# One-hot products of the last expert between two expert layers, and ten unread products moved ahead of the router's ranks

## The reference, cut to what matters

```python
# 1. gated linear attention: batch 2, 8 heads, 768 positions, head_dim 40; its output is x: 1536 tokens x 320
# 2. first expert layer: 8 experts, each token goes to its best 2 (320 -> 1024 -> 320, ReLU)
logits = x @ w_gate
noise_scale = np.log1p(np.exp(x @ w_noise))
noisy_logits = logits + noise_scale * noise
top2 = np.argpartition(-noisy_logits, 2, axis=1)[:, :2]
top2_l = np.take_along_axis(noisy_logits, top2, axis=1)
top2_w = np.exp(top2_l - top2_l.max(-1, keepdims=True))
top2_w /= top2_w.sum(-1, keepdims=True) + 1e-09
for e in range(8):
    for k in range(2):
        mask = top2[:, k] == e
        h = np.maximum(x[mask] @ w1[e], 0.0)
        out[mask] += top2_w[mask, k, None] * (h @ w2[e])
# 3. second expert layer: 4 experts, every token goes through all
p = domain_probs / (domain_probs.sum(-1, keepdims=True) + 1e-09)
for e in range(4):
    out += p[:, e:e + 1] * (np.maximum(x @ w1[e], 0.0) @ w2[e])
```

## Time and profile before

| | us |
|---|---|
| device time, median of 3 runs | 715.22 (714.48 to 716.89) |
| device time of the profiled execution | 714.77 |
| its span | 712.9 |
| TensorE busy | 680.1 (95%) |
| VectorE busy | 384.0 (54%) |
| ScalarE busy | 285.3 (40%) |
| GpSimd busy | 102.4 (14%) |

### The profile page before, as it was taken

The page is one execution under the profiler, slowest core; times in us unless marked ns, Lnnn a source line. Parts: engine busy times, 40 slices in busy tenths (PEclk is TensorE's granted clock), DMA queues, the critical chain, the costliest instruction groups (busy, mean ns, idle before and its releaser), DMA issues.

```text
span 712.9 us, 11459 instructions
## 1 busy us (share of the span) xinstructions
PE 680.1 (95%) x4265; PEld 623.2 (87%) x4265; DVE 384.0 (54%) x634; ACT 285.3 (40%) x486; POOL 102.4 (14%) x144
## 2 busy tenths in 40 slices
PE   9999989999999999997389999999999999999997
PEld 7888976999999999997388989888898898898886
DVE  6677764666644754752345545546445554454422
ACT  5545533555443654552143423324334343242311
POOL 7433202522022020000512002011100001000000
PEclk9999999999999999999599999999999999999999
DMA  6347551755544758711473425234243253332001
GB/s 226 113 112 191 192 171 38 224 164 156 168 138 128 203 156 309 265 37 39 134 225 114 130 67 166 88 111 148 88 128 88 74 146 108 108 98 65 0 0 37
DMA packets 28665, 91.85 MB, mean 129 GB/s; under 512 B 4656, under 2 KB 10800, under 8 KB 28624
## 3 DMA queue, kind: packets, MB, share of 16 engines
q1 hardware_dynamic: 21328, 75.57, 35.2%
q0 software_dynamic: 3072, 10.49, 5.1%
q10 hardware_dynamic: 4224, 5.24, 2.0%
HBM read 76.87 MB, written 14.42 MB: 128 GB/s over the span
## 4 chain that ended last, share of the span: by engine, by line
PE 91%; DVE 3%; issue 2%; DMA 2%; ACT 1%; POOL 1%; DVEq 0%; ACTq 0%; POOLq 0%
PE pY L1270 13%; PE pY L1272 13%; PE pY L1271 12%; PE pH L1255 10%; PE pH L1256 9%; PE pH L1257 9%; PE pH L1262 5%; PE pH L1260 5%; PE psYa L1142 3%; PE psD L1057 2%; PE pH L1206 2%; PE pT L1232 1%; PE psS L1077 1%; PE psYa L1162 1%; DVE PM L760 1%
## 5 line engine op out<-in xcount | busy, mean ns | idle before, releaser
L626 ACT ACTIVATE h_hi<-pH 128x512 fp32r<-128x512 f32 x160 | 95.7, 598 | 273.8 <-PE pH L1262 268.6
L947 DVE SCALAR_TENSOR_TENSOR h_lo<-pH,h_hi 128x512 fp32r<-128x512 f32 x160 | 110.5, 691 | 164.1 <-ACT h_hi L626 160.2
L1270 PE MATMUL pY<-w_hi,h_hi 128*128 128x320 f32 x608 | 189.0, 311 | 2.3 <-DVE h_lo L947 1.7
L1272 PE MATMUL pY<-w_hi,h_lo 128*128 128x320 f32 x608 | 187.5, 308 | 0.0
L1271 PE MATMUL pY<-w_lo,h_hi 128*128 128x320 f32 x608 | 187.5, 308 | 0.0
L1255 PE MATMUL pH<-x_hi,w_hi 128*128 128x512 f32 (+3 forms) x324 | 123.8, 382 | 3.7 <-issue 2.3
L746 DVE TENSOR_TENSOR w_lo<-stage,w_hi 128x1024 fp32r<-128x1024 f32 (+1 forms) x80 | 108.5, 1358 | 28.0 <-ACT w_hi L553 27.8
L1270 PEld LDWEIGHTS pY<-w_hi,h_hi 128*128 128x128 f32 x608 | 114.1, 188 | 10.4 <-issue 5.3
L1256 PE MATMUL pH<-x_lo,w_hi 128*128 128x512 f32 (+3 forms) x324 | 120.8, 373 | 0.0
L1257 PE MATMUL pH<-x_hi,w_lo 128*128 128x512 f32 (+3 forms) x324 | 120.4, 372 | 0.0
L1271 PEld LDWEIGHTS pY<-w_lo,h_hi 128*128 128x128 f32 x608 | 114.1, 188 | 3.3
(11 more groups left out here) (216 smaller groups left out, 640.3 us busy)
## 6 DMA issues: line engine op xcount, KB each, us to landing
stage<-in_w SPq DMA_DIRECT2D x40, 640.0 KB, 4.6
stage<-in_w SPq DMA_DIRECT2D x40, 512.0 KB, 3.6
stage<-in_w SPq DMA_DIRECT2D x40, 256.0 KB
results_by_slot<-acc ACTq DMA_DIRECT2D x8, 640.0 KB, 3.3
results_by_slot<-X SPq DMA_DIRECT2D x8, 640.0 KB, 8.6
qk<-in_qk_t SPq DMA_DIRECT2D x16, 240.0 KB
kv<-in_kv_n SPq DMA_DIRECT2D x8, 480.0 KB
og<-in_o_n SPq DMA_DIRECT2D x2, 960.0 KB, 6.2
```

Of the source, the lines that this page charges most:

```text
L626: act.activation(HH[s % 2][:, :], pH[s % 2][:, :], ACT.Relu).then_inc(hh_done[layer], 1)
L947: dve.scalar_tensor_tensor(out=HL[s % 2][:, :], in0=pH[s % 2][:, :], scalar=0.0, in1=f32(HH[s % 2][:, :]), op0=ALU.max, op1=ALU.subtract). ...
L1270: pe.matmul(y[:, 0:XD], hh, wh, start=(f == 0), stop=False)
L1272: return pe.matmul(y[:, 0:XD], hl, wh, start=False, stop=(f == NF - 1))
```

## The change

Two edits.

1. **Results of visit 7 don't go through DRAM for the first block.** At the end of visit 7 ScalarE copies the four `pY` tiles to `y_hi` (in `xrows[1]`) and VectorE takes the rest into `y_lo` (in the four `h` tiles). TensorE multiplies them by one-hot tiles `sel_t` (slot by token, 128x512 for each of the four slot tiles, made by VectorE during visits 2 and 3): 32 products of 128x320, eight for each token tile, into `pH` and `pT`. ScalarE scales each token tile by the weight of the last expert (`w_last`) into `XB`. The gathers from DRAM for the first block no longer wait for visit 7, only for visits 0 to 6, and read from positions `near`, in which a token's place in the last expert is replaced by its other one with weight 0 (`w_rest`). VectorE adds the two gathered results of all four tiles first, then splits both halves; TensorE turns both halves into six banks (`pS`) and then does the two half steps of `up`. ScalarE still stores the results of visit 7 for the later blocks; the zeroed slots in `results_by_slot` start one visit earlier (nine transfers of zeros for eight), so that no slot of visit 7 is undefined when it is read with weight 0. ScalarE's and VectorE's loops over visits 2 to 7 are written out.
2. **Ten unread products move**: `idle_work(16)` ahead of the ranks becomes 26, and `idle_work(22)` behind them becomes 12.

```diff
@@ gpsimd, between the layers
-            pool.wait_ge(rt_dest, 1)
-            pool.wait_ge(layer1_out, 1)
+            pool.wait_ge(near_placed, 1)
+            pool.wait_ge(ys_clear, 16 * (V1 - MUST + 1))
+            for q in range(2):
+                pool.wait_ge(ys_out[q], 16 * (MUST // 2 - q) + OUT_CREDIT)
             for hb in range(2 * BLOCKS):
                 if hb == 2:
+                    pool.wait_ge(rt_dest, 1)
+                    pool.wait_ge(layer1_out, 1)
                     pool.wait_ge(x2_ready, 4)
@@ scalar, end of visit 7
+                if last:
+                    for n in range(ST):
+                        act.activation(y_hi[:, n, :], pY[n][:, 0:XD], ACT.Copy).then_inc(yh_done, 1)
                 act.wait_ge(ys_out[q], 16 * j + OUT_CREDIT)
                 for tt in range(2):
+                    if last:
+                        act.wait_ge(yl_done, tt + 1)
                     act.activation(acc[q][:, tt, :], pY[tt][:, 0:XD], ACT.Copy).then_inc(y_copied[0], 1)
...
+            def weigh_last(tt):
+                act.wait_ge(last_mm, tt + 1)
+                act.activation(XB[:, tt, :], last_bank[tt][:, 0:XD], ACT.Copy, scale=w_last[:, tt:tt + 1]).then_inc(last_out, 1)
@@ vector
+            def slot_numbers():
...
+            def pick_slots(tiles):
+                dve.wait_ge(tails, 3)
+                for n in tiles:
+                    r = slice(0, min(P, KEPT - n * P))
+                    dve.tensor_scalar(sel_t[r, n, :], numbers[r, :], row_no[r, n:n + 1], filled[r, n:n + 1], ALU.is_equal, ALU.mult).then_inc(sel_made, 1)
...
-            visit1(0, 0, 0, chores=spare_visits)
-            visit1(1, 0, 1, chores=token_places)
-            with dve.Fori(1, MUST // 2) as j:
-                visit1(2 * j, j, 0)
-                visit1(2 * j + 1, j, 1, j < MUST // 2 - 1)
+            chores = {0: {STEPS - 1: (spare_visits,)},
+                      1: {STEPS - 3: (slot_numbers,), STEPS - 1: (token_places,)},
+                      2: {STEPS - 3: (lambda: pick_slots((0, 1)),), STEPS - 1: (near_places,)},
+                      3: {STEPS - 3: (lambda: pick_slots((2, 3)),), STEPS - 1: (near_weights,)}}
+            for v in range(MUST):
+                visit1(v, v // 2, v % 2, last=v == MUST - 1, chores=chores.get(v, {}))
...
             dve.wait_ge(layer1_mm, 1)
-            for hb in range(2):
-                mix_half(hb, 2 * hb, hb, reused=False)
-                prep(1, hb, 0, hb * HALF)
+            for tt in range(BT):
+                near_1, near_2 = (t[:, tt % 2, :] for t in near_G[tt // 2])
+                dve.wait_ge(last_out, tt + 1)
+                dve.wait_ge(gathered[tt // 2][tt % 2], 32)
+                dve.scalar_tensor_tensor(out=near_1, in0=near_1, scalar=w_rest[:, 0, tt:tt + 1], in1=XB[:, tt, :], op0=ALU.mult, op1=ALU.add).then_inc(mix, 1)
+                dve.wait_ge(mix, tt + 1)
+                dve.scalar_tensor_tensor(out=XB[:, tt, :], in0=near_2, scalar=w_rest[:, 1, tt:tt + 1], in1=near_1, op0=ALU.mult, op1=ALU.add).then_inc(x2_ready, 1)
@@ tensor
-            idle_work(16)
+            idle_work(26)
             pe.wait_ge(rt_assign, 1)
...
-            idle_work(22)
+            idle_work(12)
@@ tensor, behind visit 7
+            pe.wait_ge(sel_made, ST)
+            for tt in range(BT):
+                for n in range(ST):
+                    r = slice(0, min(P, KEPT - n * P))
+                    for m, y in enumerate((y_hi[:, n, :], y_lo[n])):
+                        if tt == 0:
+                            pe.wait_ge((yh_done, yl_done)[m], n + 1)
+                        ins = pe.matmul(last_bank[tt][:, 0:XD], sel_t[r, n, tt * P:(tt + 1) * P], y[r, :], start=(n + m == 0), stop=(n + m == ST))
+                ins.then_inc(last_mm, 1)
             pe.wait_ge(rt_tiles, 2)
             used = pe.value_load(counts[0:1, 0:1], min_val=MUST, max_val=V1)
             with pe.If(used > MUST):
@@ tensor, begin of layer 2
-            pe.wait_ge(layer1_out, 1)
...
-            pe.wait_ge(x2_ready, 2)
-            prep(1, 0, xrows[0])
+            pe.wait_ge(last_out, BT)
...
+            for half in range(2):
+                pe.wait_ge(x2_ready, 2 * half + 2)
+                for k in range(3):
+                    for n in range(2):
+                        ins = turn(pS[half][k][:, n * P:(n + 1) * P], XB[:, 2 * half + n, :], k)
+                    ins.then_inc(tr_mm[1], 1)
             pe.wait_ge(wl_done[1], PIECES + 3)
             pe.wait_ge(xl_done[1], 3)
             up(1, 0, 0, 0, HALF, inc=False)
-            pe.wait_ge(x2_ready, 4)
-            prep(1, 1, xrows[1], (0, 1))
             up(1, 1, 0, 0, HALF, inc=False)
-            prep(1, 1, xrows[1], (2,))
```

More of the change, by code:

```diff
@@ L253, in build @@
         cf = sb("cf", [1, 1])
+        numbers = sb("numbers", [P, BLOCK])
+        sel_t = sb("sel_t", [P, ST, BLOCK], F32R)
+        row_no, filled = (sb(n, [P, ST]) for n in ("row_no", "filled"))
+        free_to = sb("free_to", [P, 1])
+        of_last, of_rest, place, part_of = (sb(n, [P, 2, BT]) for n in ("of_last", "of_rest", "place", "part_of"))
+        w_rest, w_last2 = (sb(n, [P, 2, BT]) for n in ("w_rest", "w_last2"))
+        w_last = sb("w_last", [P, BT])
+        near = sb("near", [P, 2, BT], U32)
+        near_G = ((G1, G2), (X[:, 4:6, :], X[:, 6:8, :]))
+        XB = X[:, 8:12, :]
+        y_hi = xrows[1][:, :, :].bitcast(F32R)
+        y_lo = [t[:, 0:XD] for t in (HH[0], HH[1], HL[0], HL[1])]
         moe_ps = ExitStack()
@@ L285, in pair_of_results @@
         def pair_of_results(hb):
-            return (acc[1][:, 0:2, :], acc[1][:, 2:4, :]) if hb == 1 else (G1, G2)
+            return near_G[1] if hb == 1 else near_G[0]
         @block.sync
@@ L363, in _ @@
             sp.wait_ge(zeros, 1)
-            for v in range(MUST, V1):
+            for v in range(MUST - 1, V1):
                 sp.dma_start(ys[v * SLOT:(v + 1) * SLOT, :].rearrange("(p r) d -> p (r d)", p=P),
@@ L520, in _ @@
                         pool.indirect_dma_start(out=G[:, tt, :], out_offset=None, in_=ys,
[L521 removed]
+                                                in_offset=bass.IndirectOffsetOnAxis(ap=(dest if hb >= 2 else near)[:, k, t:t + 1], axis=0)).then_inc(gathered[hb == 1][tt], 16)
                 if hb in (4, 5):
@@ L676, in _ @@
                             store_results(2 * j + q, q)
+                for q in range(2):
+                    act.wait_ge(ys_out[q], 8 * used + OUT_CREDIT)
+                act.sem_inc(spares_out, 1)
+            act.sem_inc(wh_done[1], PIECES)
+            act.wait_ge(layer1_mm, 1)
+            for half in range(2):
+                c = slice(half * HALF, (half + 1) * HALF)
+                for k in range(3):
+                    act.wait_ge(tr_mm[1], 3 * half + k + 1)
+                    src = pS[half][k]
+                    r = slice(0, P) if k < 2 else slice(0, HB)
+                    act.activation(XH[0][r, k, c], src[r, 0:HALF], ACT.Copy).then_inc(xh_done[1], 1)
+                    if k == 2:
+                        act.activation(XC[0][HB:P, c], src[HB:P, 0:HALF], ACT.Copy).then_inc(xh_done[1], 1)
             for q in range(2):
@@ L948, in hidden, with visit1 @@
                                          op0=ALU.max, op1=ALU.subtract).then_inc(hl_done[layer], 1)
-            def visit1(v, j, q, another=None, chores=None):
+            def visit1(v, j, q, last=False, chores={}):
                 for s in range(STEPS):
@@ L954, in visit1 @@
                         split_lo(0, 1 - q, v + 1, (s,))
-                    if s in ROUNDS1 and another is None:
+                    if s in ROUNDS1 and not last:
                         prep(0, v + 1, 1 - q, 0, ROUNDS1[s])
-                    elif s in ROUNDS1:
-                        with dve.If(another):
-                            prep(0, v + 1, 1 - q, 0, ROUNDS1[s])
-                    if s == STEPS - 1 and chores is not None:
-                        chores()
+                    for chore in chores.get(s, ()):
+                        chore()
                 dve.wait_ge(y_mm[0], step(v, STEPS - 1) + 1 + YMM_CREDIT)
+                if last:
+                    for n in range(ST):
+                        dve.wait_ge(yh_done, n + 1)
+                        dve.tensor_tensor(y_lo[n], pY[n][:, 0:XD], f32(y_hi[:, n, :]), ALU.subtract).then_inc(yl_done, 1)
                 dve.wait_ge(ys_out[q], 16 * j + OUT_CREDIT)
```

84 lines of the change are left out of this document (58 added, 26 removed).

## The result

| | before | after |
|---|---|---|
| median of 3 runs, us | 715.22 (714.48 to 716.89) | 709.77 (709.59 to 710.64) |
| profiled execution, its span, us | 714.77, 712.9 | 709.77, 707.8 |
| ratio to before, 95% interval | | 0.993 [0.991, 0.995] |

A forecast was written before the change was run, and what follows sets the result against it. TensorE was taken as the bound, busy 680.1 of 712.9 us, its idle and half-clock time winnable. 714.77 - 1.85 (router) - 7.7 (between the layers) = 705.2, by the median 705.7; stated 705.5, range 700.3 to 709.8.

The forecast's parts named there:

- Router: Unread products around `A`: moving ten starts the last inversion group at 111.85 instead of 113.72, 1.85 us gained.
- Written-out visits, chores: Visits 2 to 7: VectorE's new chores delay a following `h_lo` by 0.5 us at most, covered by 2.1 us of lead.
- The branch on the path: Between the layers: mixing waits for `layer1_mm` behind TensorE's `counts` load (336.5) and spare-visits branch, until 341.0.
- The branch's length: TensorE's branch over the spare visits, between the layers: 3.6 us, from 3.621 in the trace before.
- list of what costs nothing: Items expected free: VectorE's chores, two `acc` copies, ninth zeros transfer, later visit 7 store, second weights near 338 instead of 352.
- One-hot products: Between the layers: 25 products left after `y_lo`, 0.147 us each, end at 340.3; last scaled token tile at 340.8.
- Mixing: VectorE between the layers: eight steps in 4.25 us, from 341.0 to 345.3.
- Clock: Between the layers TensorE's clock falls; the half steps' 16 products take 0.21 us each, 3.4 us, to 350.0.
- a second stop for code: Rival, behind the branch between the layers: another 3.6 us ahead of `layer1_mm`, 709.1 us; chance 12%.
- The other rivals: Clock holds 703.9 (15%), router without gain 707.3 (7%), slower from code stops 718.8 (4%), no effect 714 (4%).
- The branch is not in the way: Rival between the layers: branch takes 0.1 to 0.2 us or issues early; gain 12.6 + 1.85, 700.3 us; chance 13%.

The follow-up runs named there:

- a2: The changed kernel with the unread products back at 16 and 22, so the one-hot path alone: 711.61 us, 0.9957 of before.
- c2: c1 with all one-hot-path products 128 rows deep, slots beyond the 32 kept ones multiplied by 0: 703.26 us, 0.9835 of before.
- a3: The changed kernel with the loads of layer 2's second weights also waiting for `layer1_mm`: 707.96 us, 0.9898 of before.
- a4: a3 with the store of visit 7 also issued behind `layer1_mm`: 707.16 us, 0.9911 of before.
- b1: The changed kernel without TensorE's branch and its code of the spare visits, load of `counts` kept: 707.32 us, 0.9892 of before.
- c1: b4 with the wait for visit 7's store moved from ScalarE to GpSimd, which zeroes the first accumulator ahead of it: 708.02 us, 0.9889 of before.
- b4: b3 with b2's edit added: 707.75 us, 0.9916 of before.
- b3: The changed kernel with the load of `counts` and the branch ahead of the one-hot products, which stand in both arms: 708.65 us, 0.9917 of before.
- b2: The changed kernel with VectorE's wait for `layer1_mm` moved behind its eight mixing steps: 708.27 us, 0.9911 of before.

## Why the prediction was right in direction and wrong in size

- **Router: right.** 1.85 us forecast; 1.98 in the last group's start, 1.81 in layer 1's last product. `A` is read 0.28 us after the products end (0.5 forecast), the clock holds. It holds in 102 to 104 in all 14 traces with 26 and 12 products, and falls there in both with 16 and 22 (before, a2). The reason given for it, that a wait of 1.3 us did not cost the clock in 120 to 122, is weaker than it looked: at that place c2 lost it behind a wait of 1.33 us.
- **Written-out visits, chores: right**, they cost nothing. From the last inversion group to layer 1's last product it is 220.27 us after, 220.10 before; no stop for code, one more packet.
- **The branch on the path: right; its start, wrong.** The prediction let the load run "when the last wait for `y_lo` is passed", 25 products ahead of the last. The sequencer ran 15 ahead; the load came 4.65 us after the last product of layer 1, not 2.7. That is **1.9 us**. The row that the prediction read, the load at 332.3, had 11 products of layer 1 still to start, not 25.
- **The branch's length: wrong, and the largest term.** "This branch took 3.621 us" was carried over to a place where the DMA queues are full. The prediction had what fills them in its list of what costs nothing: "The second weights of layer 2 start near 338 instead of 352", and the later store beside it. They start at 335.19 and 336.81, ahead of the branch, and it takes 6.86: **3.3 us**. a3 and a4 take the length back to 5.08 and 3.32.
- **One-hot products:** "25 x 0.147" left out the change of rows; the last scaled tile ends 8.4 us after layer 1's last product instead of 7.0. It costs nothing here, since the mixing waits for the branch until 12.4.
- **Mixing: right**, 4.3 us for eight steps (4.25).
- **Clock: nearly right.** It fell, as forecast, but came back at 351.9, amid the half steps: from the mixing's end to `down` it is 6.8 us instead of 7.6, **0.8 us** to the good.

The step that failed is thus the one on the branch: its length and its start were put 5.2 us too small together. 1.9 + 3.3 - 0.8 = 4.4 us; the profiled execution (709.77) is 4.6 above the 705.2 worked out for it. The measured time is that of the rival "a second stop for code" (709.1), but its mechanism is not what happened: there is one stop, and one packet in it, which comes late behind other transfers. The other rivals' mechanisms did not show in the changed kernel. "The branch is not in the way" put the first `down` at 348.0, 14.2 us after the last product's start; b1 is that case and has 18.8, since the wait for the store of visit 7 stands there (3.7 us of TensorE's time), so its 700.3 was too low by more than 4 us. The measured time stands at the range's upper end: 709.77 is 0.03 inside it, 0.993 of 715.22 is 710.2 and outside.

The Trainium skill, "Runtime: NRT & Kernel Launch", section Instruction fetch mechanics, says that a taken branch outside the window stalls until the code is fetched. The runs agree: no kernel with the branch passed it in under 3.3 us, and 7.5 was the longest.

## What to carry to other kernels

A duration in a trace holds for what ran beside it: a branch to unfetched code that costs 3.6 us on quiet DMA queues costs 5 to 7 behind a store and weight loads. When a change makes a transfer early, list what else uses the queues in the time it moves into, the engines' own code among it, and not only who reads the transfer. Put a run-time branch where the queues are quiet and the engine has products queued, and look at the wait that it leaves behind: behind one of 2.55 us c1 lost the clock and came to 21.7 us, behind one of 2.32 b4 held it and came to 18.7. One profile of a kernel does not tell what its clock does in the next execution.

## What the runs showed of the hardware that was not expected

- One branch over the same code took 3.30 to 3.80 us in the eight kernels in which its packet ran on quiet queues, 5.08 behind a store of 640 KB, and 6.32 to 7.46 in the six executions with this store and weight loads beside it. The packet of code ran 1.0 to 1.4, 2.8, and 3.8 to 5.0 us after its start, and in all 15 the branch ended 2.3 to 2.6 us after the packet's start.
- TensorE products of 320 columns that follow one with another number of rows (128 and 32) start 0.25 us behind it, those that keep it 0.147.
- The clock fell behind waits of 2.36, 2.55 and 2.33 us in b3, c1 and c2, and held behind one of 2.32 in b4. The length of the wait did not settle it at shorter ones either. Ahead of the first visit it fell in c2 behind 1.33 us (121.8) and held in the changed kernel and in b1 behind 1.32. In a4 and b2 it fell amid the one-hot products, 3.4 and 3.6 us after layer 1's last product and behind a wait of 0.62, where seven other executions with the same wait held it. Times of one kernel lie up to 7 us apart (c1: 701.76 to 709.08); that the clock makes this spread is argued, not shown.
- The store of visit 7 landed 11.3 us after its issue beside the weights, 4.1 without them.
